# High, low and one-hot rows of the attention operands written in place by the engines instead of placed by DMA, and the product with the values in one burst

## The reference

```python
q_bits = (np.einsum('bhsd,dk->bhsk', q, proj) > 0).astype(np.int64)
k_bits = (np.einsum('bhsd,dk->bhsk', k, proj) > 0).astype(np.int64)
mask = q_bucket[:, :, :, None] == k_bucket[:, :, None, :]
scores = scale * np.matmul(q, k.transpose(0, 1, 3, 2))
scores = np.where(mask, scores, -1000000000.0)
attn = np.exp(scores - np.max(scores, axis=-1, keepdims=True))
attn = attn / (np.sum(attn, axis=-1, keepdims=True) + 1e-09)
out = np.matmul(attn, v)
# then x = _moe_ref(x): five-tap gate, x @ w_val, gated, @ w_out
# then _moe2_ref(x): token mix, relu(xk @ w_k)**2 @ w_v, gated by sigmoid(xr @ w_r)
```

## Time and profile before

| | us |
|---|---|
| median of 3 runs (lowest, highest) | 552.98 (550.57, 557.4) |
| the profiled execution | 550.8 |
| its span, first to last instruction | 549.0 |
| mean granted PE clock | 0.981 |
| PE busy | 488.2 (89%) |
| DVE, ACT, POOL busy | 341.4, 255.5, 190.6 |

### The profile page before, as it was taken

How to read it: one execution, slowest core, us unless ns; L and a number is a source line. 1 busy time by engine, 2 the same in 40 slices (tenths; PEclk the granted TensorE clock), 3 DMA queues, 4 the chain that set the end, 5 groups by cost and what they waited for, 6 DMA issues and landing times.

```text
span 549.0 us, 9293 instructions
## 1 busy us (share of the span) xinstructions
PE 488.2 (89%) x3504; PEld 409.9 (75%) x3504; DVE 341.4 (62%) x596; ACT 255.5 (47%) x569; POOL 190.6 (35%) x202
## 2 busy tenths in 40 slices
PE   2499999999979899998897969899899899899998
PEld 0376665666656566665666959799899899899997
DVE  2286776766657666669959778538738729634311
ACT  3186756656565555756523452252352342344140
POOL 3060604214050320605014352552752643544240
PEclk9999999999999899999999799899999899999999
DMA  8958465665956549480400000100100100000101
GB/s 220 206 115 246 94 184 135 153 170 111 233 107 175 126 105 238 101 204 3 169 1 0 1 0 1 40 2 1 40 1 0 41 1 1 20 21 0 39 2 39
DMA packets 20813, 45.98 MB, mean 84 GB/s; under 512 B 3744, under 2 KB 8864, under 8 KB 20768
## 3 DMA queue, kind: packets, MB, share of 16 engines
q1 hardware_dynamic: 20768, 45.38, 33.5%
HBM read 17.06 MB, written 3.15 MB: 37 GB/s over the span
## 4 chain that ended last, share of the span: by engine, by line
PE 45%; DVE 26%; DMA 9%; SPq 8%; issue 5%; ACT 5%; POOL 1%; DVEq 0%; ACTq 0%
PE ps L585 23%; DVE gate L730 10%; DMA k<-hot_k 8%; PE ps L538 8%; PE ps L573 7%; SPq L206 7%; PE ps L549 5%; DVE tmp_a L816 3%; DVE gate L727 2%; DVE tmp_b L814 2%; DVE tmp_b L819 2%; DVE x L721 2%; ACT pt L384 2%; DVE negmax L691 2%; ACT probs L376 1%
## 5 line engine op out<-in xcount | busy, mean ns | idle before, releaser
L691 DVE TENSOR_REDUCE negmax<-ps 128x1 f32<-128x768 f32 x96 | 91.7, 956 | 74.5 <-PE ps L538 73.4
L538 PE MATMUL ps<-k,q 128*128 128x384 f32 x384 | 95.0, 370 | 19.4 <-DMA k<-hot_k 10.9
L538 PEld LDWEIGHTS ps<-k,q 128*128 128x128 f32 x384 | 64.7, 193 | 53.7 <-issue 27.2
L376 ACT ACTIVATE probs<-ps,negmax 128x768 f32<-128x768 f32 x96 | 86.5, 901 | 36.4 <-DVE negmax L691 34.5
L549 PE MATMUL ps<-ident,probs 128*128 128x128 f32 x576 | 81.4, 277 | 1.9 <-DVE pt L698 1.9
L573 PE MATMUL ps<-pt,vals 128*64 128x384 f32 x384 | 72.5, 500 | 5.4 <-DVE x L721 5.4
L549 PEld LDWEIGHTS ps<-ident,probs 128*128 128x128 f32 x576 | 68.5, 142 | 9.7 <-issue 2.7
L384 ACT ACTIVATE pt<-ps 128x384 f32<-128x384 f32 x96 | 46.9, 489 | 49.1 <-PE ps L549 49.0
L730 DVE SCALAR_TENSOR_TENSOR gate<-x,conv_sb,gate 128x256 f32<-128x256 f32 x96 | 59.7, 622 | 3.2
L284 POOL COPY rcp_w<-rcp 128x384 f32<-128x384 f32 x16 | 8.1, 507 | 151.0 <-DVE rcp L714 151.0
L585 PE MATMUL ps<-xk_hi,w_hi 128*128 128x256 f32 x192 | 54.9, 286 | 5.1 <-POOL xr_lo L334 5.1
(11 more groups left out here) (84 smaller groups left out, 1063.3 us busy)
## 6 DMA issues: line engine op xcount, KB each, us to landing
k<-k_hi SPq DMA_DIRECT2D x32, 192.0 KB, 3.8
q<-q_hi SPq DMA_DIRECT2D x32, 192.0 KB, 4.0
w_raw<-w SPq DMA_DIRECT2D x8, 640.0 KB, 8.4
raw_q<-qT SPq DMA_DIRECT2D x8, 384.0 KB, 3.3
raw_k<-kT SPq DMA_DIRECT2D x8, 384.0 KB, 5.5
vals<-v SPq DMA_DIRECT2D x16, 192.0 KB, 2.9
k<-k_lo SPq DMA_DIRECT2D x16, 192.0 KB, 4.1
q<-q_lo SPq DMA_DIRECT2D x16, 192.0 KB, 4.6
```

What stands on the lines that cost most here:

```text
L376: act.activation(probs[par][:, :], score[par], ACT.Exp, bias=negmax[:, t:t + 1], accum_out=sums[:, t:t + 1]).then_inc(exp_done, 1)
L538: last = pe.matmul(ps[:, 2 * par + half, 0:HALF], qq[h][:, q], kk[h][:, half * HALF:(half + 1) * HALF], start=first, stop=not first)
L691: dve.tensor_reduce(negmax[:, t:t + 1], score[g % 2], AX.XY, ALU.max, negate=True).then_inc(max_done, 1)
```

## The change

The eight transfers per head are gone, with q_hi, q_lo, k_hi, k_lo, hot_q, hot_k as tensors of their own. There are three sets of q1, k1, q2, k2, used in turn by head number, and every engine writes straight into the rows of a set, across the halves where needed. So a step that was one instruction on 128 partitions for the pair becomes instructions on 64 partitions per head: two casts of keys per head on DVE, two scaled copies of queries per head on ACT (one goes to q1, one to q2), one-hot rows per head, low parts per head on POOL. The scaled query in full precision (q_eighth) is made by POOL instead of ACT. The bit codes are cast by POOL instead of DVE, and ACT's queue issues the three small first loads.

The order within a pair moves: project from t = 0 to 1, matches from t = 3..6 to 4..7, spread and reciprocals_up from tt = 4 to 2, and both now stand ahead of the transposes and copies of their tile. The product of the previous head is one burst of six key tiles at tt = 3, ahead of the transposes. normalise moves to tt = 5 of the next head (before: tt = 0 of the head after that).

```diff
-R_STEP = 4
-PV_STEPS = {1: (0, 1), 3: (2, 3), 5: (4, 5)}
-MATCH_STEPS = (3, 4, 5, 6)
+R_STEP = 2
+PV_STEPS = {3: tuple(range(KT))}
+MATCH_STEPS = (4, 5, 6, 7)
+SETS = 3
...
             def reload_qk(p):
-                sp.wait_ge(klo_done, p)
-                sp.wait_ge(qlo_done, p)
+                sp.wait_ge(qhi_done, 4 * p)
+                sp.wait_ge(qscaled, p)
                 sp.wait_ge(bits_mm, p)
...
+                sp.wait_ge(khi_done, 4 * p)
+                sp.wait_ge(klo_done, 2 * p)
...
+            def low_keys(head):
+                rows, n = (LO, HI)[head % 2], head % SETS
...
+                pool.wait_ge(khi_done, 2 * head + 1)
+                wait(pool, s_done, KT * (head - SETS + 1))
+                pool.tensor_tensor(k1[n][HI, :], raw_k[rows, :], k2[n][rows, :], ALU.subtract).then_inc(klo_done, 1)
...
+            def high_queries(head, second):
+                rows, n = (LO, HI)[head % 2], head % SETS
+                act.wait_ge(q_in, 16 * (head // 2 + 1))
+                wait(act, s_done, KT * (head - SETS + 1))
+                to = (q1[n][HI, :], q2[n][LO, :])[(head + second + 1) % 2]
+                act.activation(to, raw_q[rows, :], ACT.Copy, scale=DH ** -0.5).then_inc(qhi_done, 1)
...
-                first_half_up(g)
                 if tt == R_STEP and head:
                     reciprocals_up(head - 1)
+                first_half_up(g)
                 if i < LAST:
-                    if t == 1:
-                        high_queries(i + 1)
-                    if t == 2:
-                        scale_queries(i + 1)
+                    if t in (0, 1):
+                        high_queries(2 * i + 2, t)
                     if t in (MATCH_STEPS[0], MATCH_STEPS[2]):
-                        hot_queries(i + 1, MATCH_STEPS.index(t) // 2)
+                        for h in range(2):
+                            hot_queries(i + 1, MATCH_STEPS.index(t) // 2, h)
+                    if t in (5, 7):
+                        high_queries(2 * i + 3, (t - 5) // 2)
...
-            for j in range(4):
+            for j in (0, 1, 3, 2):
                 match(0, j)
...
-                transposes(g)
                 if tt == R_STEP and head:
                     spread(head - 1)
+                if tt in PV_STEPS and head:
+                    product(head - 1, PV_STEPS[tt])
+                transposes(g)
                 if i < LAST:
-                    if t == 0:
+                    if t == 1:
                         project(i + 1)
...
+            def high_keys(head):
+                rows, n = (LO, HI)[head % 2], head % SETS
+                dve.wait_ge(k_in, 16 * (head // 2 + 1))
+                wait(dve, s_done, KT * (head - SETS + 1))
+                for part in ((LO, HI), (HI, LO))[head % 2]:
+                    dve.tensor_copy(k2[n][part, :], raw_k[rows, :]).then_inc(khi_done, 1)
...
                 second_half_up(g)
-                if tt == 0 and head >= 2:
-                    normalise(head - 2)
+                if tt == KT - 1 and head:
+                    normalise(head - 1)
                 if i < LAST:
                     if t == 1:
-                        high_keys(i + 1)
+                        high_keys(2 * i + 2)
                     if t == 2:
                         bits_out(i + 1)
                     if t in (MATCH_STEPS[1], MATCH_STEPS[3]):
-                        hot_keys(i + 1, MATCH_STEPS.index(t) // 2)
+                        for h in range(2):
+                            hot_keys(i + 1, MATCH_STEPS.index(t) // 2, h)
+                    if t == 6:
+                        high_keys(2 * i + 3)
```

More of the change, by code:

```diff
@@ L49, in turns0, with match_count, hot_count @@
 def turns0(head, tt):
-    return KT * head + tt + max(0, head - 1) + (1 if head >= 1 and tt > R_STEP else 0)
+    return KT * head + tt + max(0, head - 1) + (1 if head >= 1 and tt >= R_STEP else 0)
+def match_count(p, j):
+    return 4 * p + ((0, 1, 3, 2).index(j) if p == 0 else j) + 1
+def hot_count(head):
+    if head == 0:
+        return 2
+    return 4 * (head // 2) + 3 + head % 2
 def turn_r(head):
@@ L57, in turn_r @@
         return turns0(NHEADS, 0)
-    return turns0(head + 1, R_STEP) + 1
+    return turns0(head + 1, R_STEP) - 1
 def build(nc, qT, kT, v, proj, w1, w2, conv, mu_k, mu_r, codes, out):
@@ L80, in build @@
         raw_k = sb("raw_k", [P, SEQ], F32, att)
[L81 to L90, removed]
+        q_eighth = sb("q_eighth", [P, SEQ], F32, att)
+        q1, k1, q2, k2 = [{} for _ in range(4)]
+        for n in range(SETS):
+            s = (NHEADS + n) % SETS
+            q1[s] = sb(f"q1_{s}", [P, SEQ], F32R, att)
+            k1[s] = sb(f"k1_{s}", [P, SEQ], F32R, att)
+            q2[s] = sb(f"q2_{s}", [P, SEQ], F32R, att)
+            k2[s] = sb(f"k2_{s}", [P, SEQ], F32R, att)
         vals = [sb(f"vals{h}", [P, KT, DH], F32, att) for h in range(2)]
@@ L233, in load_w @@
                 sp.dma_start(w_raw[:, :], w1[p, :, :]).then_inc(w_in, 16)
-            load_qk(0)
-            sp.wait_ge(proj_zero, 1)
-            for h in range(2):
-                sp.dma_start(proj_bd[DH * h:DH * h + DH, BITS * h:BITS * h + BITS], proj).then_inc(proj_in, 16)
-            sp.dma_start(codes_f[:, :, :], codes).then_inc(codes_in, 16)
+            sp.dma_start(raw_q[:, :], qT[0, :, :]).then_inc(q_in, 16)
+            sp.dma_start(raw_k[:, :], kT[0, :, :]).then_inc(k_in, 16)
             load_v(A, 0)
@@ L306, in _ @@
                                base=0, pattern=[[-1, P]], channel_multiplier=1).then_inc(ident_up, 1)
-            low_parts(0)
+            scale_queries(0)
+            pool.wait_ge(codes_in, 16)
+            pool.tensor_copy(codes_b[:, :, :], codes_f[:, :, :]).then_inc(codes_up, 1)
+            pool.wait_ge(codes_up, 1)
+            for head in range(2):
+                low_keys(head)
+                low_queries(head)
+            pool.wait_ge(qlo_done, 2)
             for i in range(PAIRS):
@@ L616, in _ @@
                     s_val_tile(0, 2 * (t % 2) + 1)
-                if tt in PV_STEPS and head:
-                    product(head - 1, PV_STEPS[tt])
             spread(NHEADS - 1)
@@ L777, in _ @@
                         dve.wait_ge(x_done, x_ready(0))
-                        for h in range(2):
-                            dve.wait_ge(placed[h], PAIRS * PLACED)
+                        dve.wait_ge(s_done, KT * (NHEADS - 2))
                         dve.wait_ge(consts_in, 48)
@@ L786, in _ @@
             add_eps(NHEADS - 1)
-            dve.wait_ge(pv_done, NHEADS - 1)
             reciprocals(NHEADS - 1)
-            normalise(NHEADS - 2)
             def gated(c, m):
```

150 lines of the change are left out of this document (72 added, 78 removed).

## The result

| | before | after |
|---|---|---|
| median of 4 runs of each (lowest, highest) | 551.78 (543.38, 557.4) | 558.21 (556.71, 561.41) |
| profiled execution, its span | 550.8, 549.0 | 556.71, 554.9 |
| mean granted PE clock | 0.981 | 0.985 |

The ratio is 1.018, with a 95% interval of 1.012 to 1.024: the change costs some 2%. The forecast was 556.

What follows compares the result with a forecast made beforehand. PE, 92% busy, was taken as the bound. Start -8.0, pair 0 +1.0, six pairs +10.8 and last stretch +1.5 summed to +5.3 on 550.8: 556 us, with 538 to 572 for 8 in 10.

Steps and rivals of the forecast that it cites:

- start: Up to the first scores: they run at 10.2 instead of 20.5, part goes back; -8.0 us (between -6 and -10.3).
- pair 0: First pair, with no product or normalise in its first half: +1.0 us.
- six pairs: The six full pairs: 34.0 us each against 32.2, +1.8 per pair, +10.8 in all; bounds 29.8 and 36.
- last stretch: Last stretch, where the taps make DVE slowest and the two bursts stop it twice: +1.5 us (0 to +5).
- dense part: The dense part, 262.34 us, is not touched by the change: 0.
- the steps of the layout: One pair laid out tile by tile from trace pitches, time 0 after the burst at t = 3: 6.4 us of waits.
- The 28.0: PE's work per pair in us: 29.6, with -1.84 from fewer turns and the burst, half given back by new turns.
- The old waits: PE's waits per pair for the placement, for normalise (0.68) and before the spread (2 x 0.34): all go.
- the 2.3 counted back: At the start, DVE's 3.83 us idle for keys, less 1.5 of cover, leaves about 2.3 of reload wait.
- the stalls hide: Rival: PE stays the bound, pairs of 29.8, 529 to 530 us (540 half-way); chance 0.2 for below 542.
- casts on DVE wait for POOL: Rival: each second key cast stands for POOL's subtraction, pairs of 36 to 36.5, 571 us; chance 0.25.
- The third rival: The start gains less, 3 us instead of 8, through dearer low parts or a longer reload wait: 561; chance 0.1.

Runs made afterwards that it cites:

- The half bursts: The kernel after with the product in two bursts of three key tiles at tt = 1 and 4 instead of one burst: 542.24 us in one execution.
- split rows: The kernel before with k_hi, q_hi and both one-hot rows each written by two 64-partition instructions, placement kept: 569.3 us, ratio 1.031.
- the spread at tt = 4: The kernel after with three product pieces, one-hot keys ahead of normalise, loads on SP, spread behind transposes at tt = 4 instead of 2: 539.34 us, ratio 0.979.

## Why the prediction was right, and where it was not

The sum came out at +5.3, measured +5.9 between the spans. By its steps, with the scores at t = 3 as the bounds in the attention part:

| step | forecast | measured |
|---|---|---|
| start | -8.0 | -7.0 |
| pair 0 | +1.0 | +3.8 |
| six pairs | +10.8 | +11.3 |
| last stretch | +1.5 | +1.3 |
| dense part | 0 | -3.5 |

The mechanism is right, but the close agreement of the totals is in part luck: in the attention part +5.3 was forecast and +9.4 measured, and the scatter of the dense part took 3.5 of it back.

**The pairs were right, as a sum and place by place.** 34.0 was forecast and 33.9 measured. The waits, by the steps of the layout: at t = 4 for the exponential 0.7 (measured 0.68); the third match 0.9 (0.67); t = 7 the second transposes 0.5 and the exponential 0.3 (0.36 and 0.19); t = 8 for the reciprocals 1.5 (1.45); t = 1 for the copy 1.3 (1.04); t = 2 0.9 (0.68). With 0.3 of small waits that did not come it was 6.4 against 5.07. PE's work was 28.8 and not 28.0, and the two errors cancel. The 28.0 does not follow from its own terms: 29.6 less 1.84 is 27.8, and with half of the gain given back, as it says itself, 28.6 to 28.7. With that and the 6.4 of waits the pair would have been 35. That 34.0, chosen between 33.5 and 34.4, came out within 0.1 is therefore better than the working deserved. The old waits went, as said.

**Its reason for the waits was wrong in one point.** "Their copies wait for transposes that come behind the burst": with the burst behind the transposes the same seven waits came. What holds is the other half: without pieces beside the late steps PE's work per tile does not cover DVE's and ACT's queues. The half bursts took away just the waits at tt = 1 and behind it, and the burst put alone into the kernel before cost 16 us between the spans.

**The start was mis-sized.** "5.3 + 1 + 2 x 1.81 + 0.2" had POOL free to cast the codes at 5.3. The scaling held it to 5.98, and the codes landed at 7.97, so the scores came at 12.63, not 10.2. With the loads on SP they came at 11.03. From the end of the last low part to the scores it took 0.4, where I had 0.2. Of the 2.3 counted back only 0.9 came (first scores to t = 3: 12.36 for 11.44), so at t = 3 the start was 1.0 short and not 2.4.

**Pair 0 was the worst term:** +3.8 for +1.0. PE's busy time is the same as before (26.16 for 26.15), so the whole 3.8 is idle time, 4.98 for 1.23: the waits of a full pair mostly came here too, where the forecast had counted little. Within the busy time the clock has a part: after the wait of 1.44 at 37.95 PE's granted clock was 0.61 on average for about 4 us (0.50, the level of 1.2 GHz, from 38 to 40; otherwise up to the full 2.4 GHz), which by itself is 4.1 x 0.39 = 1.6 us of a full clock's work. The same trace shows that price: from the spread at t = 8 to the one at t = 2 of the next pair it took 18.35 us here and 16.9 in the pairs that follow, at the full clock. Stretches of after:

```profile
33.00:37.90 4.90, 2.83 (x18) 2.21 (x17) 4.76 (x8) 4.70 (x10) 4.31 (x3) 0.98 0.33 127
37.90:42.00 4.10, 4.05 (x18) 2.99 (x20) 1.51 (x2) 1.48 (x3) 0.07 (x1) 0.61 0.00 0
```

Ahead of the fall PE had worked only 2.83 of 4.90 us. The last stretch came as forecast; in it the transposes waited once 2.21 for DVE's copy, as the burst stopped DVE.

**The dense part** was 3.5 us shorter with the same instructions. The profiles of the twelve experiments, in which it is the same too, have it between 258.9 and 261.2 us; 262.3 before and 258.8 after are the two ends of this scatter. The clock does not explain it: over the whole part it reads 0.97 in both.

**The rivals.** That the stalls hide did not come: a pair of 33.9 is far from 29.8. Even without the burst and with the spread behind, the pair was 32.1. That casts on DVE wait for POOL is seen in one place only, where the scaling runs beside them. The third row has all casts of the run (least, median and longest in ns):

```profile
120.28 2.31 POOL L254 TENSOR_SCALAR q_eighth<-raw_q 128x768 f32<-128x768 f32 x1
...
121.37 1.63 DVE L735 CAST k<-raw_k 64x768 fp32r<-64x768 f32 x2
...
L735 DVE CAST k<-raw_k x32: 540/557/1061, 5.7 to 240.0; 64x768 fp32r<-64x768 f32 x32
```

The two casts take 1.63 for 1.15 at 103.63 above, +0.5 per pair on DVE, all of it in the second: the first, begun 1.09 us into the scaling, takes 0.54, the second, from 121.94, 1.06, and it ends 0.41 behind POOL's end at 122.59. By the prediction's own sign, casts that last over 1 us, this one counted against it; it cost PE nothing that the rows show, since the maximum behind it is followed by the burst. The Trainium skill, SBUF — State Buffer, section Who interferes with whom, would let casts in the two-port mode stand until the scaling is over, and then last 1.22 + 1.15 = 2.4; the trace does not agree for the pair of casts, with 1.63, nor for the first. The place that the rival had named is the other one, where the low keys begin beside the second cast. There DVE came first, as the forecast had argued, the casts kept their 1.15, and POOL's step took 2.14 at 104.32 for 1.80 at the start.

The third rival, a start that gains less, was right in kind: the first scores were 2.4 us late, of which 1.0 was left at t = 3, where it had named 5.

**Left open.** Why the placement's wait differs so much from pair to pair and run to run (543 to 565 us for the kernel before), why it grew with split rows, and how much the spread at tt = 4 lost by itself. The changed places of the projection, the matches and normalise were not undone one by one, so their share in the pairs is not known.

## What to carry to other kernels

A matrix product that PE could do at any time is also the cover under which the other engines catch up: put its pieces right ahead of the steps whose inputs come late, and count what a burst takes away from there before counting the turns it saves. Removing a transfer pays only as far as the schedule around it is kept; here the whole was a loss of 1.8%, and with two of its parts undone it was a gain of 1.5% (3.3% with the one-hot keys and the loads in a better order too). A hand layout of one period from the pitches between neighbours in the trace found each wait within 0.3 us; it was worst in pair 0, which it did not lay out, and where the landing of a load came in. A difference of a few us between two profiles can come from a part that nobody changed: compare it stretch by stretch, between the same steps.

## What the runs showed of the hardware that I had not expected

ACT loses its overlap between neighbours too. ACT in the kernel after, one-hot queries and a cast of one half between a copy and an exponential:

```profile
96.91 0.49 ACT L394 ACTIVATE pt<-ps 128x384 f32<-128x384 f32 x1
97.40 1.18 ACT L378 ACTIVATE q<-ps,neg_two 64x384 fp32r<-64x384 f32 x2
98.61 0.90 ACT L386 ACTIVATE probs<-ps,negmax 128x768 f32<-128x768 f32 x1
...
100.00 0.85 ACT L407 ACTIVATE q<-raw_q 64x768 fp32r<-64x768 f32 x1
100.88 0.90 ACT L386 ACTIVATE probs<-ps,negmax 128x768 f32<-128x768 f32 x1
```

A one-hot row of one half has a pitch of 0.605 (98.61 less 97.40, halved) where whole rows had 0.46, the cast 0.88 where the whole one had 0.75, and the copy ahead of it 0.49 for 0.37: about 0.13 at each turn to another set of partitions, on ACT as on DVE (0.59 for 0.47 there, where I had counted 0.08).

POOL's scaling of 128x768 by a constant takes 2.13 to 2.37, more than its subtraction of two such inputs (1.81), and a subtraction on 64 partitions (1.80) as much as one on 128.

The granted clock fell behind some gaps on PE and not behind others of the same kind. It fell to an average of 0.61 in the kernel after (above), to 0.57 for 4 us in the kernel before, behind a wait of 1.84 at 188.31, and with split rows to 0.64 from 135.60 to 140.30, after the wait of 2.58 shown above; with the burst alone it read 0.50 for 5 us behind a wait of 3.04 at 163.14. It stayed full behind the wait of 2.49 in the earlier trace rows and, with the burst alone, behind one of 2.79 at 129.06. So the length of the wait alone does not tell them apart. What does was not tried.
